# A Fourier stage in fp32 hi/lo products: even and odd columns apart, half of the outputs by matmul

## The reference

```python
def _moe2_ref(x, w_ch1, w_ch2) -> np.ndarray:
    X = np.fft.fft(x, axis=1)
    X = np.fft.fft(X, axis=2)
    mixed = np.real(X).astype(np.float32)
    u = x + mixed
    mu = np.mean(u, axis=-1, keepdims=True)
    var = np.mean((u - mu) ** 2, axis=-1, keepdims=True)
    un = (u - mu) / np.sqrt(var + 1e-06)
    ch = np.maximum(un @ w_ch1, 0.0) @ w_ch2
    return (u + ch).astype(np.float32)
```

## Time and profile before

| | us |
|---|---|
| runs | 571.97 median of 3 (571.94, 571.97, 574.22) |
| the profiled execution | 572.5, of which the span is 570.7 |
| TensorE busy in the span | 560.2 (98%), weight loads 498.7 (87%) |
| VectorE busy | 362.2 (63%) |
| ScalarE busy | 253.0 (44%) |
| GpSimd busy | 250.6 (44%) |

### The profile page before, as it was taken

How to read it: one execution, slowest core, us unless ns; L and a number is a source line. 1 busy time by engine, 2 the same in 40 slices (tenths; PEclk the granted TensorE clock), 3 DMA queues, 4 the chain that set the end, 5 groups by cost and what they waited for, 6 DMA issues and landing times.

```text
span 570.7 us, 9580 instructions
## 1 busy us (share of the span) xinstructions
PE 560.2 (98%) x3592; PEld 498.7 (87%) x3592; DVE 362.2 (63%) x634; ACT 253.0 (44%) x510; POOL 250.6 (44%) x275
## 2 busy tenths in 40 slices
PE   7999999999999999999999999999999999999997
PEld 5889887998989999899888888998989898998996
DVE  3975968676643796376989954769873634344333
ACT  2565324655643454434463533354554334434420
POOL 2664236366634454204676542147563332333311
PEclk8999999999999999999999999999999999999999
DMA  8980201412322120211112211121222212221142
GB/s 303 360 345 3 77 34 42 151 58 74 94 74 69 63 73 22 73 56 53 41 56 74 75 45 48 57 66 27 75 74 75 74 61 70 74 74 56 38 148 111
DMA packets 24014, 49.11 MB, mean 86 GB/s; under 512 B 2328, under 2 KB 3488, under 8 KB 23968
## 3 DMA queue, kind: packets, MB, share of 16 engines
q1 hardware_dynamic: 23376, 46.65, 24.2%
q0 software_dynamic: 448, 1.71, 1.0%
q10 hardware_dynamic: 144, 0.13, 0.1%
HBM read 45.34 MB, written 3.15 MB: 85 GB/s over the span
## 4 chain that ended last, share of the span: by engine, by line
PE 86%; DVE 9%; issue 2%; ACT 1%; DMA 1%; SPq 0%; DVEq 0%; ACTq 0%
PE banks L1147 14%; PE banks L1148 14%; PE banks L1146 14%; PE banks L1419 11%; PE banks L1421 11%; PE banks L1422 11%; PE banks L1212 2%; PE banks L1200 2%; PE banks L1171 1%; PE banks L1256 1%; PE banks L1188 1%; DVE sums L736 1%; DVE u L907 1%; DVE al L736 1%; PE banks L1276 1%
## 5 line engine op out<-in xcount | busy, mean ns | idle before, releaser
L363 POOL TENSOR_TENSOR w2l<-raw,w2h 128x512 fp32r<-128x512 f32 x56 | 74.6, 1333 | 154.1 <-ACT w2h L478 154.1
L1419 PE MATMUL banks<-th,al 128*128 128x384 f32 x392 | 131.9, 337 | 1.1 <-DVE tl L736 0.4
L1421 PE MATMUL banks<-tl,ah 128*128 128x384 f32 x392 | 132.2, 337 | 0.0
L1422 PE MATMUL banks<-th,ah 128*128 128x384 f32 x392 | 132.0, 337 | 0.0
L478 ACT ACTIVATE snap<-banks 128x384 f32<-128x384 f32 x84 | 41.1, 489 | 126.5 <-PE banks L1422 126.4
L736 DVE TENSOR_TENSOR al<-raw,ah 128x512 fp32r<-128x512 f32 (+1 forms) x112 | 87.4, 801 | 6.1 <-ACT ah L478 5.1
L1032 DVE TENSOR_TENSOR snap<-banks,snap 128x384 f32<-128x384 f32 x84 | 46.4, 552 | 65.0 <-PE banks L1422 64.5
L1419 PEld LDWEIGHTS banks<-th,al 128*128 128x128 f32 x392 | 73.6, 188 | 9.4 <-issue 1.3
L1421 PEld LDWEIGHTS banks<-tl,ah 128*128 128x128 f32 x392 | 73.5, 188 | 6.0
L1422 PEld LDWEIGHTS banks<-th,ah 128*128 128x128 f32 x392 | 73.6, 188 | 0.0
L363 POOL TENSOR_TENSOR raw<-raw 128x256 f32<-128x256 f32 x84 | 69.3, 841 | 2.2
(11 more groups left out here) (171 smaller groups left out, 908.3 us busy)
## 6 DMA issues: line engine op xcount, KB each, us to landing
raw<-w1b_dram SPq DMA_DIRECT2D x16, 512.0 KB, 3.3
raw<-w2b_dram SPq DMA_DIRECT2D x32, 256.0 KB, 2.9
raw<-w1a_dram SPq DMA_DIRECT2D x12, 512.0 KB, 3.3
raw<-w2a_dram SPq DMA_DIRECT2D x24, 256.0 KB, 3.3
kTs<-kT_dram SPq DMA_DIRECT2D x8, 384.0 KB, 6.6
qTs<-qT_dram SPq DMA_DIRECT2D x8, 384.0 KB, 7.3
vns<-vn_dram SPq DMA_DIRECT2D x8, 384.0 KB, 5.6
kns<-kn_dram SPq DMA_DIRECT2D x8, 384.0 KB, 7.6
```

The costliest lines, as they stand in the source:

```text
L363: return nc.gpsimd.tensor_tensor(o, i0, i1, ALU.subtract)
L1419: mm(o[:, 0:HALF], al[:, a, cols], th[b][:, t, k, :], start=start and k == 0, stop=False, skip_group_check=True)
L1421: mm(o[:, 0:HALF], ah[:, a, cols], tl[b][:, t, k, :], start=False, stop=False, skip_group_check=True)
L1422: last = mm(o[:, 0:HALF], ah[:, a, cols], th[b][:, t, k, :], start=False, stop=(k == 1), skip_group_check=True)
```

## The change

The stationary operand of the second stage (columns j of the first stage's result) is now ordered by the parity of j: the folds write their 256 columns as 128 even and then 128 odd ones, so tile k = 0 holds even j and tile k = 1 odd j. The constants are loaded to match (row 2p + k on partition p, plane k), and only their first 130 columns (k = 0 to 128 and a pad). In a bank the sum over even j goes to columns 0 to 129 and that over odd j to columns 130 to 259; they are no longer added by TensorE. The number of matmuls stays, each has 130 columns instead of 258. VectorE makes P - Q and P + Q over 260 columns (`dsub`, `dadd`), and `spread` forms from each the outputs k = 0 to 128 (even plus odd) and, written backwards, k = 256 down to 129 (even minus odd). A semaphore `y_halves` stands between these and the adds to the residual. The edge row is first copied from the bank and then spread in the same way.

```diff
+NQ = DM // 4 + 2
...
+        dsub, dadd = misc[:, 0:2 * NQ], misc[:, 2 * NQ:4 * NQ]
...
-            qs[b] = sb(work, f"qs{b}", [L, 2, NK2])
+            qs[b] = sb(work, f"qs{b}", [L, 2, 2 * NQ])
...
-        p_read = sem("dft2_p_read")
+        p_read, y_halves = sem("dft2_p_read"), sem("dft2_halves_ready")
...
-        consts = [(c1, c1h, c1l, NA, NK1), (s1, s1h, s1l, NA, HALF), (c2, c2h, c2l, 2, NK2), (s2, s2h, s2l, 2, NK2)]
+        consts = [(c1, c1h, c1l, NA, NK1), (s1, s1h, s1l, NA, HALF), (c2[:, 0:NQ], c2h, c2l, 2, NQ),
+                  (s2[:, 0:NQ], s2h, s2l, 2, NQ)]
...
-                    pool.dma_start(cview(j), consts[j][0].rearrange("(k p) n -> p k n", p=L)).then_inc(s_craw, 16)
+                    pool.dma_start(cview(j), consts[j][0].rearrange(("(k p) n -> p k n", "(p k) n -> p k n")[j // 2], p=L)).then_inc(s_craw, 16)
...
-                copy(qs[b][:, a % 2, :], src[:, 0:NK2]).then_inc(q_ready, 1)
+                copy(qs[b][:, a % 2, :], src[:, 0:2 * NQ]).then_inc(q_ready, 1)
...
+            def by_parity(x):
+
+                return x.rearrange("p (m r) -> p r m", r=2)
+
+            def parted(x):
+                return x.rearrange("p (r m) -> p r m", r=2)
+
             def fold_even(b, a):
 
                 n, i = NA * b + a, (NA * b + a) % 2
@@ -919,14 +929,15 @@
                 link(nc.vector.tensor_tensor(ssum[:, 0:DM], u[:, NC * b + a, :], u[:, NC * b + NA + a, :], ALU.add))
                 if a == 2:
                     dve.wait_ge(eh_ready, n - 1)
-                nc.vector.tensor_tensor(eo[b][:, i, 0:FH], ssum[:, 0:FH], ssum[:, DM:FH:-1], ALU.add)
+                nc.vector.tensor_tensor(parted(eo[b][:, i, 0:FH]), by_parity(ssum[:, 0:FH]),
+                                        by_parity(ssum[:, DM:FH:-1]), ALU.add)
                 nc.vector.tensor_copy(eo[b][:, i, FH:FH + 1], ssum[:, FH:FH + 1])
 
             def fold_odd(b, a):
                 n, i = NA * b + a, (NA * b + a) % 2
                 dve.wait_ge(dif_ready, n + 1)
-                nc.vector.tensor_tensor(eo[b][:, i, FH + 1:DM + 1], sdif[:, 0:FH], sdif[:, DM:FH:-1],
-                                        ALU.subtract).then_inc(eo_ready, 1)
+                nc.vector.tensor_tensor(parted(eo[b][:, i, FH + 1:DM + 1]), by_parity(sdif[:, 0:FH]),
+                                        by_parity(sdif[:, DM:FH:-1]), ALU.subtract).then_inc(eo_ready, 1)
...
             def row_sum(b):
                 dve.wait_ge(rr_ready, b + 1)
-                nc.vector.tensor_tensor(rsum[:, 0:FH], rraw[:, 0:FH], rraw[:, DM:FH:-1], ALU.add)
+                nc.vector.tensor_tensor(parted(rsum[:, 0:FH]), by_parity(rraw[:, 0:FH]), by_parity(rraw[:, DM:FH:-1]),
+                                        ALU.add)
                 nc.vector.tensor_copy(rsum[:, FH:FH + 1], rraw[:, FH:FH + 1]).then_inc(rs_ready, 1)
...
-            K = FH + 1
+            K, KQ = FH + 1, FH // 2 + 1
+
+            def spread(o_low, o_high, x, rows):
+
+                even, odd = x[rows, 0:NQ], x[rows, NQ:2 * NQ]
+                nc.vector.tensor_tensor(o_low[rows, 0:KQ], even[:, 0:KQ], odd[:, 0:KQ], ALU.add)
+                return minus(o_high[rows, FH:FH - KQ + 1:-1], even[:, 0:KQ - 1], odd[:, 0:KQ - 1])
 
             def dft_add(b, a, p):
 
                 n = NA * b + a
                 ua, ub = u[:, NC * b + a, :], u[:, NC * b + NA + a, :]
+                everywhere = slice(0, L)
                 dve.wait_ge(q_ready, n + 1)
                 dve.wait_ge(p_done, 4 * b + a + 1)
                 if a:
                     dve.wait_ge(y_added, 4 * b + a)
-                nc.vector.tensor_tensor(ym[b][:, 0:K], p[:, 0:K], qs[b][:, a % 2, 0:K], ALU.subtract)
-                nc.vector.tensor_tensor(yp[b][:, 0:K], p[:, 0:K], qs[b][:, a % 2, 0:K], ALU.add).then_inc(p_read, 1)
+                minus(dsub, p[:, 0:2 * NQ], qs[b][:, a % 2, :])
+                nc.vector.tensor_tensor(dadd, p[:, 0:2 * NQ], qs[b][:, a % 2, :], ALU.add).then_inc(p_read, 1)
                 dve.wait_ge(p_read, n + 1)
+                spread(ym[b], yp[b], dsub, everywhere)
+                spread(yp[b], ym[b], dadd, everywhere).then_inc(y_halves, 1)
+                dve.wait_ge(y_halves, 4 * b + a + 1)
                 nc.vector.tensor_tensor(ua[:, 0:K], ua[:, 0:K], ym[b][:, 0:K], ALU.add)
                 nc.vector.tensor_tensor(ua[:, K:DM], ua[:, K:DM], yp[b][:, FH - 1:0:-1], ALU.add)
                 nc.vector.tensor_tensor(ub[:, 0:K], ub[:, 0:K], yp[b][:, 0:K], ALU.add)
@@ -982,9 +1004,12 @@
 
                 dve.wait_ge(p_done, 4 * b + 4)
                 dve.wait_ge(y_added, 4 * b + NA)
-                row = u[0:1, NC * b + NA, :]
-                nc.vector.tensor_tensor(row[:, 0:K], p[0:1, 0:K], rraw[:, 0:K], ALU.add)
-                nc.vector.tensor_tensor(row[:, K:DM], p[0:1, FH - 1:0:-1], rraw[:, K:DM], ALU.add).then_inc(y_added, 1)
+                row, one = u[0:1, NC * b + NA, :], slice(0, 1)
+                link(nc.vector.tensor_copy(dsub[one, :], p[one, 0:2 * NQ]))
+                spread(ym[b], ym[b], dsub, one).then_inc(y_halves, 1)
+                dve.wait_ge(y_halves, 4 * b + 4)
+                nc.vector.tensor_tensor(row[:, 0:K], ym[b][one, 0:K], rraw[:, 0:K], ALU.add)
+                nc.vector.tensor_tensor(row[:, K:DM], ym[b][one, FH - 1:0:-1], rraw[:, K:DM], ALU.add).then_inc(y_added, 1)
...
-            def mm3(o, lh, ll, rh_, rl_, start, stop):
-
-                mm(o, ll, rh_, start=start, stop=False)
-                mm(o, lh, rl_, start=False, stop=False)
-                return mm(o, lh, rh_, start=False, stop=stop)
+            def mm3(o, lh, ll, rh_, rl_, start, stop, **kw):
+
+                mm(o, ll, rh_, start=start, stop=False, **kw)
+                mm(o, lh, rl_, start=False, stop=False, **kw)
+                return mm(o, lh, rh_, start=False, stop=stop, **kw)
...
-                for k in range(2):
-                    mm3(o[:, 0:NK2], tph[b][:, k, cols], tpl[b][:, k, cols], c2h[:, k, 0:NK2], c2l[:, k, 0:NK2],
-                        k == 0, False)
-
-                last = mm(o[:, 0:NK2], tehl[b][:, cols], e1r[:, W1PAD:W1PAD + NK2], start=False, stop=True)
+                mm3(o[:, 0:NQ], tph[b][:, 0, cols], tpl[b][:, 0, cols], c2h[:, 0, 0:NQ], c2l[:, 0, 0:NQ],
+                    True, False, skip_group_check=True)
+                mm(o[:, 0:NQ], tehl[b][:, cols], e1r[:, W1PAD:W1PAD + NQ], start=False, stop=True, skip_group_check=True)
+                last = mm3(o[:, NQ:2 * NQ], tph[b][:, 1, cols], tpl[b][:, 1, cols], c2h[:, 1, 0:NQ], c2l[:, 1, 0:NQ],
+                           False, True, skip_group_check=True)
                 last.then_inc(p_done, 1)
...
                 cols = slice(a * L, (a + 1) * L)
                 for k in range(2):
-                    last = mm3(o[:, 0:NK2], tqh[b][:, k, cols], tql[b][:, k, cols], s2h[:, k, 0:NK2], s2l[:, k, 0:NK2],
-                               k == 0, k == 1)
+                    last = mm3(o[:, k * NQ:(k + 1) * NQ], tqh[b][:, k, cols], tql[b][:, k, cols], s2h[:, k, 0:NQ],
+                               s2l[:, k, 0:NQ], k == 0, True, skip_group_check=True)
                 last.then_inc(q_done, 1)
```

## The result

The median of the changed kernel is 575.79 us (4 runs, 575.12 to 576.61) beside 572.37 for the kernel before (4 runs, 571.94 to 574.22): ratio 1.0046, 95% interval 1.0026 to 1.0066. The same kernel run again as a control on another occasion, beside 35 runs of the kernel before (median 573.32), gave 575.17 (12 runs), ratio 1.0015 (0.9996 to 1.0035). A ratio is the recorded estimate with its interval and not the quotient of the two medians, which is 1.0060 and 1.0032. The intervals overlap; both estimates put the change on the slow side, by 0.46% and 0.15%, and the second cannot be told from no change. The forecast was 574.4 us, +0.43%.

What follows compares the result with a forecast made beforehand. TensorE was taken to bound the kernel (86% of the chain). A12's waits of +2.98 us less 0.52 for shorter matmuls gave +2.46, so 574.4 us (+0.43%) on the 571.97 median; 8-in-10 range 572.0 to 583.3.

Steps and rivals of the forecast that it cites:

- what decides: Second stage: A12, next product in the edge's bank, waits for dft_edge's later end; margins 1.35 and 1.26 us; +2.98 us together.
- the load's pace: P and Q matmuls: loading 128 stationary columns allows one matmul per 0.11 us; a unit of seven takes 0.77 us.
- the gain per matmul: P and Q matmuls: 0.01 us saved each; the 52 ahead of the wait give -0.52 us.
- VectorE's additions: Second stage: added operations cost 0.92 us per dft_add unit and 0.97 us in dft_edge, with backward writes at no extra cost.
- the wait in batch 1: A12 in batch 1: dft_edge ends 2.76 us later, A12 moves from 370.97 to 372.52; with the load +1.66 us.
- the open load: A12 after its wait: its first weights are loaded in the open, 0.11 us more.
- B: P and Q matmuls: narrow fp32r runs at the plain fp32 rate, 0.24 us each, +11.0 us, 583.0 us; chance 0.25.
- C: Folds: reading every second element costs an element time, 1.88 us in batch 1 and 1.55 in batch 0; 577.8 us; chance 0.08.
- D: P and Q matmuls: loads do not pace, columns only, 0.06 us saved each; 571.9 us; chance 0.13.
- the change halves TensorE's part: Second stage: 92 x 0.06 = 5.5 us saved, 566.5 us, needing D and a VectorE chain within 1.3 us; chance 0.02.

Runs made afterwards that it cites:

- The two single parts: Changed kernel with VectorE's bank work as before, only TensorE's part: 573.03 us; kernel before plus VectorE's added operations alone, into scratch: 575.54 us.
- the released bank: Changed kernel, with A12 waiting for the copy of the edge row out of the bank instead of the end of dft_edge: 572.75 us, ratio 0.9988.
- the 66 columns: Changed kernel with only 66 of the 130 moving columns in each P and Q matmul, the rest not computed: 576.48 us.

## Why the prediction was right or wrong

**Right: what decides.** VectorE's added operations end dft_edge later than A12 wants its bank, and the narrow matmuls are worth too little to pay for it. The two single parts (-0.7 and +2.7 us) and the released bank (-2.6) show each half of this by itself.

**Right: the load's pace.** Forecast 0.11 us a matmul, found 0.11. The unit was 0.72 us from its start to the next step's and not 0.77: the first narrow matmul takes only 0.05. Its own load had run beside the wide matmul ahead (250.46), the second load starts with it (250.69), and each further matmul starts 0.05 or 0.06 behind the start of its load. The wide matmul behind the unit starts as close behind its load, and takes 0.29 us instead of 0.23 or 0.24 (251.41 to 251.70). From the unit's start to the second wide matmul it is 1.01 us, and was 1.08 before: 0.07 saved by seven.

**Mis-sized: the gain per matmul.** I took 0.01 us from the rounded 0.12 and 0.11. It is about 0.008 (0.7 over 92). The sum also counted P unit 1 twice, once among the 26 matmuls a batch and once as 0.05 us on VectorE's side; A12 waits for VectorE, so only the second belongs there, and it was 0.12: VectorE starts 1.09 us behind the unit's first matmul (251.78 - 250.69) and not 1.21. The 19 ahead of P unit 1 gained 0.14 us a batch (from Q unit 0's start to P unit 1's in batch 0: 15.89 to 15.75), 0.28 together. The forecast had -0.52.

**Right: VectorE's additions.** Forecast 0.92 and 0.97, found 0.93 and 0.97. Writing backwards and contention with GpSimd cost nothing here.

**Mis-sized: the wait in batch 1.** Forecast 1.21 us in batch 0 and 1.55 in batch 1; A12 came 9.67 - 8.50 = 1.17 and 9.68 - 8.50 = 1.18 later. The step that failed read dft_add(2)'s start in batch 1 (366.64) as what the new operations would be added to. It held 0.35 us of late start that belonged to the old stream of instructions and vanished in the new one: dft_add(2) came 369.36 - 364.71 = 4.65 us behind its P unit, in batch 0 255.33 - 250.69 = 4.64.

**Right: the open load.** 260.36 to 260.65 is 0.29 us where the step was 0.17 before: +0.12 each, forecast 0.11.

**The sum again, from what was measured:** 1.17 + 1.18 + 2 x 0.12 - 0.28 = +2.31 us; the late part says +2.2; forecast +2.46. That the sum came so near is in part luck, since two wrong sizes partly cancelled: waits 0.41 us too long together (0.37 of it in batch 1) and a gain 0.24 us too large. The rest of the distance from 574.4 to the median of 575.79 is, as far as is known, scatter: 0.40 us of it is in the kernel before (572.37 instead of 571.97), and the early part, which differed by up to 1.5 us between two executions of the same changed kernel, can hold the rest, though only profiled executions show it. In the larger comparison the medians are 1.85 us apart (575.17 and 573.32).

**The range and the chances.** The range of 572.0 to 583.3 us was stretched to reach B, so that the result lies in it says little; it also lies in the forecast's own 573.3 to 576.6. The likeliest single value, +0.43%, was near the 0.46% measured, but 0.55 of the chances lay on more than 0.5%, and neither the recorded ratios nor the late part's 0.38% went that far.

**The rivals.** B, the slower rate for narrow fp32r, fell: units of 0.72 us, not 1.7. C, the cost of a stride, fell: the folds did not move. D, columns alone, fell by the 66 columns. That the change halves TensorE's part fell with D.

## What to carry to other kernels

Before halving a matmul's moving columns, look at the interval between two weight loads: from 258 columns down, with a full load for each, half the columns were worth about 0.008 us a matmul here, and the operations that put the output together again cost another engine much more. When work is added to the engine that hands a bank back, find the first product that takes that bank and its margin (1.35 us here against 2.5 added), and release the bank at the last read of it rather than at the end of what follows: one copy's semaphore took back 2.6 us. A start read from the trace may hold a delay that is not the work's; compare the same step in the other batch before building on it.

## What the runs showed of the hardware that was not expected

- A VectorE instruction waiting on TensorE started 0.35 us later (1.56 instead of 1.21 us behind the same matmul) at one place in its instruction stream; 4 or 16 tiny instructions ahead removed it. The cause is open.
- The first fp32r matmul of a narrow run takes 0.05 us by its record and so about 0.05 less than the load's pace of 0.11, and the wide one behind the run about 0.05 more (0.29 us): the load's cost moves by one matmul to the end.
- A matmul of 130 columns with 64 stationary columns takes 0.06 us a step: half the stationary columns make the load cheap enough for 130 columns to run near their own pace (0.053 us, estimated from 0.41 ns a column).
- After one pause of 2.10 us on TensorE the granted clock fell to 0.50 from about 260.8 to 264.1 us, which cost 1.5 us. The same pause in the other batch of that execution, and the pauses of 1.1 to 1.3 us in the other kernels, left it at 1.00.
